# Clustered attention and two mixers on one core: mask rows of the first pair transposed early, transfers issued by SyncE, the other mask rows in eight pieces

## What is computed

```python
q_assign = np.argmax(np.einsum('bhsd,hcd->bhsc', q_n, c_n), axis=-1)
k_assign = np.argmax(np.einsum('bhsd,hcd->bhsc', k_n, c_n), axis=-1)
mask = q_assign[:, :, :, None] == k_assign[:, :, None, :]
scores = scale * np.matmul(q, k.transpose(0, 1, 3, 2))
scores = np.where(mask, scores, -1000000000.0)
attn = softmax(scores)
out = np.matmul(attn, v)
x = _moe_ref(x=out as (batch, token, head*dim), **moe_kwargs)
return _moe2_ref(x=x, **moe2_kwargs)
```

## Time and profile before

| | us |
|---|---|
| median of 3 runs | 792.31 (790.92 to 794.45) |
| the profiled execution | 793.93 |
| its span, first to last instruction | 792.0 |
| PE busy | 768.9 (97%) |
| DVE busy | 448.5 (57%) |
| ACT busy | 359.4 (45%) |
| POOL busy | 136.2 (17%) |
| preparation, to the last turning-back | 0 to 45 |
| first pair's tiles | 45 to 75 |
| rest of attention | 75 to 269 |
| mixers | 269 to 792 |

### The profile page before, as it was taken

The page is one execution under the profiler, slowest core; times in us unless marked ns, Lnnn a source line. Parts: engine busy times, 40 slices in busy tenths (PEclk is TensorE's granted clock), DMA queues, the critical chain, the costliest instruction groups (busy, mean ns, idle before and its releaser), DMA issues.

```text
span 792.0 us, 12875 instructions
## 1 busy us (share of the span) xinstructions
PE 768.9 (97%) x3985; PEld 661.3 (83%) x3985; DVE 448.5 (57%) x761; ACT 359.4 (45%) x740; POOL 136.2 (17%) x162
## 2 busy tenths in 40 slices
PE   6979999999999789999999999999999999999998
PEld 6968999999999668888888888888888888888886
DVE  4758999999999684333532353334254335334333
ACT  5547888888888524323332332332123233323321
POOL 1341332233228660000300040000300000000000
PEclk9979999999999999999999999999999999999999
DMA  8725444444441223332333323333003233332334
GB/s 289 184 82 135 111 105 119 104 120 102 121 101 49 74 87 93 105 98 87 97 90 106 89 83 119 84 101 96 11 1 107 93 93 92 95 106 84 102 105 174
DMA packets 82712, 81.08 MB, mean 102 GB/s; under 512 B 7296, under 2 KB 68864, under 8 KB 82688
## 3 DMA queue, kind: packets, MB, share of 16 engines
q1 hardware_dynamic: 81984, 79.00, 34.9%
q10 hardware_dynamic: 704, 1.77, 0.6%
HBM read 56.95 MB, written 4.72 MB: 78 GB/s over the span
## 4 chain that ended last, share of the span: by engine, by line
PE 63%; DVE 2%; ACT 0%; issue 0%
PE bank L958 29%; PE bank L967 29%; PE bank L945 2%; PE bank L926 2%; PE bank L909 1%; DVE kT_hi L1068 1%; DVE x L1086 0%; DVE x L1119 0%; DVE w_lo L1058 0%; DVE t L1077 0%; ACT qT_hi L1017 0%; DVE uT_lo L1063 0%
## 5 line engine op out<-in xcount | busy, mean ns | idle before, releaser
L1095 DVE SCALAR_TENSOR_TENSOR h_lo<-bank,h_hi 128x512 fp32r<-128x512 f32 x84 | 58.0, 691 | 259.3 <-ACT h_hi L1036 259.3
L1036 ACT ACTIVATE h_hi<-bank 128x512 fp32r<-128x512 f32 x84 | 50.2, 598 | 299.1 <-PE bank L958 299.1
L958 PE MATMUL bank<-uT_hi,w_hi 128*128 128x512 f32 x336 | 131.2, 391 | 0.0
L967 PE MATMUL bank<-w_hi,h_hi 128*128 128x512 f32 x336 | 131.1, 390 | 0.0
L958 PE MATMUL bank<-uT_hi,w_lo 128*128 128x512 f32 x336 | 130.8, 389 | 0.0
L967 PE MATMUL bank<-w_hi,h_lo 128*128 128x512 f32 x336 | 130.8, 389 | 0.0
L958 PE MATMUL bank<-uT_lo,w_hi 128*128 128x512 f32 x336 | 130.7, 389 | 0.0
L967 PE MATMUL bank<-w_lo,h_hi 128*128 128x512 f32 x336 | 130.7, 389 | 0.0
L572 DVE TENSOR_TENSOR pT_lo<-back,pT_hi 128x384 fp32r<-128x384 f32 x192 | 98.1, 551 | 8.1 <-ACT pT_hi L475 4.8
L475 ACT ACTIVATE pT_hi<-back 128x384 fp32r<-128x384 f32 x192 | 84.5, 496 | 38.2 <-PE back L709 35.7
L565 DVE TENSOR_REDUCE negmax<-front 128x1 f32<-128x768 f32 x96 | 91.2, 951 | 7.9 <-PE front L618 7.9
(11 more groups left out here) (123 smaller groups left out, 1051.9 us busy)
## 6 DMA issues: line engine op xcount, KB each, us to landing
w_raw<-in_moe_w_ch_dram SPq DMA_DIRECT2D x168, 256.0 KB, 2.8
Q<-qT_hi SPq DMA_DIRECT2D x64, 96.0 KB, 2.1
K<-kT_hi SPq DMA_DIRECT2D x64, 96.0 KB, 2.1
q_raw<-in_q_dram SPq DMA_DIRECT2D x8, 384.0 KB, 6.6
k_raw<-in_k_dram SPq DMA_DIRECT2D x8, 384.0 KB, 6.4
Q<-qT_lo SPq DMA_DIRECT2D x32, 96.0 KB, 2.1
K<-kT_lo SPq DMA_DIRECT2D x32, 96.0 KB, 2.1
v_raw<-in_v_dram SPq DMA_DIRECT2D x16, 192.0 KB, 2.8
```

Source lines behind the costliest of these rows:

```text
L958: last = nc.tensor.matmul(hid[par][:, :], w[par][:, kd, :], y[cc % 2][:, kd, :], start=(kd == 0 and m == 0), stop=(kd == KD - 1 and m == 2))
L967: last = nc.tensor.matmul(acc[k][:, :], y[par][:, k * P:(k + 1) * P], w[par][:, :], start=(start and m == 0), stop=(stop and m == 2))
L1036: nc.scalar.activation(h_hi[par][:, :], hid[par][:, :], ACT.Relu).then_inc(h_hi_made, 1)
L1095: nc.vector.scalar_tensor_tensor(out=h_lo[par][:, :], in0=hid[par][:, :], scalar=0.0, in1=h_hi[par][:, :].bitcast(F32), op0=ALU.max, op1=A ...
```

## The change

- **PE, preparation:** the two OH steps go. Two steps `("OHQ", 0, u)` come, six transposes each of only the first pair's 32 one-hot rows, one behind SB(2, queries) and one behind SA(2, keys). They take part in the alternation of `back[0]` and `back[1]`. `("S", 0, 0)` goes ahead of BACK of group 3 and S(1) comes behind it; BACK 3 waits for the low part of T(7,q).
- **DVE:** the row maximum of tile 0 (`MAX`) goes behind FIRST of group 2 and ahead of BEST of group 3.
- **ACT:** copies the OHQ steps into `ohq`, issues no DMA any more.
- **First pair:** the one-hot rows of both batch entries are transposed in eight pieces, behind S(2), T(0), S(3), T(1), S(4), T(2), and two behind S(5). Each batch entry has its own place in `x`.
- **SP:** the first eight raw loads, then the wait for three low parts; then each of the other eight loads is followed by three of the 24 head rows. Then both v loads, the mask rows of the first pair from `ohq` (four DMAs), U and V, the four stores of mask rows (each behind its copies), and the loop as before.

```diff
-            ohT = [x[:, 4 + n, 0:S] for n in range(2)]
+            ohT = [[x[:, 4 - 2 * b + n, 0:S] for n in range(2)] for b in range(B)]
+            ohq = [x[0:2 * C, GT * n:GT * n + GT, S:S + S // GT] for n in range(2)]
...
-        pe_steps += [sims[LAST][0], ("BACK", LAST - 1, 0), sims[LAST][1], ("OH", 0, 0), sims[LAST][2], ("OH", 0, 1),
-                     sims[LAST][3], ("BACK", LAST, 0)]
+        for u in range(2):
+            pe_steps.insert(pe_steps.index(("SB", LAST - 1, 0) if u == 0 else ("SA", LAST - 1, 1)) + 1, ("OHQ", 0, u))
+        pe_steps += [sims[LAST][0], ("BACK", LAST - 1, 0), sims[LAST][1], sims[LAST][2], sims[LAST][3],
+                     ("S", 0, 0), ("BACK", LAST, 0), ("S", 1, 0)]
...
-        back_T = [step for step in T_order if step != in_front]
-        place = {step: back[(n + 1) % 2] for n, step in enumerate(back_T)}
+        back_steps = [step for step in pe_steps if step[0] in ("T", "OHQ") and step != in_front]
+        place = {step: back[n % 2] for n, step in enumerate(back_steps)}
...
-        dve_steps += [("BEST", LAST - 1, 0), ("EQ", LAST - 1, 0), ("FIRST", LAST - 1, 0), ("BEST", LAST, 0), ("EQ", LAST, 0)]
+        dve_steps += [("BEST", LAST - 1, 0), ("EQ", LAST - 1, 0), ("FIRST", LAST - 1, 0), ("MAX", 0, 0), ("BEST", LAST, 0), ("EQ", LAST, 0)]
-        OH_PIECES = 4
-        OH_COPIES = 2 + OH_PIECES
+        OH_PIECES = 8
+        PIECES_AFTER = {("S", 2): (0,), ("T", 0): (1,), ("S", 3): (2,), ("T", 1): (3,), ("S", 4): (4,), ("T", 2): (5,),
+                        ("S", 5): (6, 7)}
...
+            for _, i, n in T_order[0:NPAIR]:
+                load_raw(i, n)
             sp.wait_ge(prep_lo, T_place["T", 0, 1])
-            head_rows(0, 0)
-            head_rows(0, 1)
+            for at, (_, i, n) in enumerate(T_order[NPAIR:]):
+                sp.wait_ge(raw_tr, T_place["T", i - PAIRS, n])
+                load_raw(i, n)
+                for row in range(3 * at, 3 * at + 3):
+                    head_row(0, row // 12, row % 12)
+            head_v(0, 0)
+            head_v(0, 1)
+            for u in range(2):
+                sp.wait_ge(ohq_copied, u + 1)
+                for j in range(2):
+                    sp.dma_start((Q2, K2)[u][j][D:D + C, :].rearrange("p (n c) -> p n c", n=GT).bitcast(F32),
+                                 ohq[u][j * C:(j + 1) * C, :, :]).then_inc(head_in[j], 16)
...
+            for b in range(B):
+                for u in range(2):
+                    store_onehots(b, u, 4 * b + 2 * u + 2)
             sp.wait_ge(prep_lo, 2 * NPAIR)
+            sp.wait_ge(oh_stored[0], 32)
             sp.wait_ge(oh_stored[1], 32)
...
-                elif kind == "OH":
-                    act.wait_ge(oh_tr, u + 1)
-                    mask_rows(u, ohT[u], place[kind, i, u][:, 0:S])
-                    act.wait_ge(oh_copied, u + 1)
-                    for j in range(2):
-                        act.dma_start((Q2, K2)[u][j][D:D + C, :].bitcast(F32),
-                                      ohT[u][j * C:(j + 1) * C, :]).then_inc(head_in[j], 16)
-                    act.dma_start(onehot_dram[u, 0:P, :], ohT[u]).then_inc(oh_stored[0], 16)
+                elif kind == "OHQ":
+                    act.wait_ge(ohq_tr, u + 1)
+                    mask_rows(u, ohq[u], place[kind, i, u][0:2 * C, 0:S].rearrange("p (n c) -> p n c", n=GT),
+                              2 * C).then_inc(ohq_copied, 1)
...
-                    if first_pair and t in (2, 3):
-                        onehot_piece(2 * t - 3)
+                    for m in PIECES_AFTER.get(("S", t + 2), ()) if first_pair else ():
+                        onehot_piece(m)
...
-                if (kind, i, u) in back_T[2:]:
+                if (kind, i, u) in back_steps[2:]:
+                    before, at, which = back_steps[back_steps.index((kind, i, u)) - 2]
...
+                b, u, half = m // 4, m // 2 % 2, m % 2
+                pe.wait_ge(oh_made, 2 * b + 2)
+                pe.wait_ge(oh_eq, LAST + 1)
+                wait(pe, oh_copied, m)
```

More of the change, by code:

```diff
@@ L223, in attention @@
         in_front = ("T", 0, 1)
-        back_T = [step for step in T_order if step != in_front]
-        place = {step: back[(n + 1) % 2] for n, step in enumerate(back_T)}
+        back_steps = [step for step in pe_steps if step[0] in ("T", "OHQ") and step != in_front]
+        place = {step: back[n % 2] for n, step in enumerate(back_steps)}
         place[in_front] = front[:, 2 * BANK:4 * BANK]
-        place["OH", 0, 0] = place["OH", 0, 1] = back[0]
+        assert place["T", NPAIR - 1, 1] is back[0]
         def sim_place(i, u):
@@ L276, in _, with head_row, head_v @@
             v_heads = v.rearrange("b h s d -> (b h) s d")
[L278 to L287, removed]
+            def head_row(g, j, n):
+                dst, src = ((Q1[j][0:D, :], hi[0]), (Q1[j][D:P, :], lo[0]), (K1[j][0:D, :], hi[1]), (K1[j][D:P, :], hi[1]),
+                            (Q2[j][0:D, :], hi[0]), (K2[j][0:D, :], lo[1]))[n // 2]
+                e = n % 2
+                sp.dma_start(dst[:, e * GW:(e + 1) * GW].bitcast(F32),
+                             src[e * D:(e + 1) * D, g, j * GW:(j + 1) * GW].bitcast(F32)).then_inc(head_in[j], 16)
+            def head_v(g, j):
                 wait(sp, v_ready[j], g)
@@ L306, in _ @@
                 for j in range(2):
-                    head_rows(g, j)
+                    wait(sp, scored, g * TPP + (NT * (j + 1) - TPP))
+                    for n in range(12):
+                        head_row(g, j, n)
+                    head_v(g, j)
                     head_onehots(g, j)
@@ L420, in exp, with mask_rows @@
                                      accum_out=sums[:, t % TPP:t % TPP + 1]).then_inc(exp_done, 1)
-            def mask_rows(u, dst, lead):
+            def mask_rows(u, dst, lead, rows=P):
                 if u == 0:
[L425 to L428, removed]
+                    return nc.scalar.activation(dst, lead, ACT.Relu, scale=MASKED, bias=masked[0:rows, :])
+                return nc.scalar.activation(dst, lead, ACT.Sign)
             for kind, i, u in pe_steps:
@@ L493, in body @@
                     high(t, 1)
-                    if first_pair and t in (1, 2):
-                        onehot_piece(2 * t - 2)
+                    for m in PIECES_AFTER.get(("T", t), ()) if first_pair else ():
+                        onehot_piece(m)
                 if last_pair:
@@ L558, in _ @@
                                             ALU.is_equal).then_inc(oh_eq, 1)
+                elif kind == "MAX":
+                    rowmax(0, i)
                 else:
@@ L588, in body @@
                 if first_pair:
[L589 to L590 removed]
+                    rowmax(0, 1)
                     first_link(LAST)
@@ L643, in _ @@
                     continue
+                if kind == "S":
+                    if i == 0:
+                        pe.wait_ge(oh_eq, LAST)
+                    else:
+                        pe.wait_ge(sim_copied, 2 * (LAST + 1))
+                    scores(0, i)
+                    continue
                 if kind == "BACK":
                     if i == LAST:
-                        pe.wait_ge(prep_lo, T_place["T", NPAIR - 1, 1])
+                        pe.wait_ge(prep_lo, T_place["T", NPAIR - 1, 0])
                     for n in range(2):
@@ L657, in _ @@
                 out = place[kind, i, u]
-                if kind == "OH":
-                    pe.wait_ge(prep_lo, T_place["T", NPAIR - 2, 1])
-                    wait(pe, oh_copied, u)
-                elif (kind, i, u) in back_T[2:]:
-                    pe.wait_ge(prep_lo, T_place[back_T[back_T.index((kind, i, u)) - 2]])
+                if (kind, i, u) in back_steps[2:]:
+                    before, at, which = back_steps[back_steps.index((kind, i, u)) - 2]
+                    if before == "T":
+                        pe.wait_ge(prep_lo, T_place[before, at, which])
+                    else:
+                        pe.wait_ge(ohq_copied, which + 1)
                 if kind == "T":
@@ L711, in body @@
                             last.then_inc(p_tr, 1)
-                        if first_pair and n in (1, 2):
-                            onehot_piece(2 * n - 2)
                     elif kind == "AV":
@@ L738, in body @@
                         last.then_inc(av_tr, 1)
+                    for m in PIECES_AFTER.get((kind, n), ()) if first_pair else ():
+                        onehot_piece(m)
             over_pairs(pe, body)
```

56 lines of the change are left out of this document (21 added, 35 removed).

## The result

The changed kernel takes 794.53 us (median of 17 runs, 792.81 to 796.53), the kernel before 792.44 in the runs beside it (17 runs, 789.67 to 796.06). The ratio is 1.0026, 95% interval 1.0014 to 1.0037: 2.1 us slower. That is inside the 0.5% that the prediction took as no change, but clear of noise and outside the range of the prediction (787.5 to 793.8). What was named as rival C decided it: the raw loads come late.

A forecast was written before the change was run, and what follows sets the result against it. TensorE, busy 97% of the 792.0 us span, was taken as the bound. Gap 3.0, bank waits -1.0, maximum +1.3, pieces and ScalarE -1.3 sum to 2.0 us gained: median 792.31 to 790.3 us, range 787.5 to 793.8.

The forecast's parts named there:

- rival C: Preparation: late raw loads land 2.4 to 4.6 us after they are wanted; far end 794.9 us; chance 9%.
- the one on the raw loads: Preparation: held-back loads shared with head rows on SyncE's queue land in 4.4 us, so none is late.
- The gap at BACK 3: Group 3's last turning-back: TensorE's wait for ScalarE's copy goes once SyncE issues the DMAs; gain 3.0 us.
- Bank waits: Preparation: TensorE waits about 0.8 and 0.4 us for low parts before T(6,k) and T(7,k); cost 1.0 us.
- The maximum: First pair's start: row maximum 0 ahead of group 3's maximum and compare, tile 2 near 45.8; gain 1.3 us.
- Pieces and ACT: First pair, tiles 2 to 5: eight pieces and waits for ScalarE's copies give back 1.3 us.
- The second pair: Chain from the last mask piece to the second pair's first score tile unchanged; wait of about 1.5 us stays.
- Rival B: First pair: the clock falls all the same, three rounds cost 3.3 us, giving 793.6 us; chance 12%.
- a clock of 0.50 anywhere after 14 us: Sign that the forecast is wrong and the clock falls all the same.

The follow-up runs named there:

- a1: The changed kernel with SyncE issuing all 16 raw loads first and the 24 head rows after them; ratio 0.9985 to the kernel before.
- a5: a3 and a4 together, plus the row maximum of tile 0 ahead of FIRST of group 2 on VectorE; ratio 0.9974 to the kernel before.
- a2: a1 with SyncE waiting for three low parts ahead of the last eight raw loads, no head rows between them; ratio 0.9986 to the kernel before.
- b3: b2 with SyncE's wait for the landed stores right ahead of each later pair's mask rows; 787.5 us, ratio 0.9930 to the kernel before.
- a3: a1 with VectorE making T(7,q)'s low part ahead of the maximum and compare of group 1; ratio 0.9972 to the kernel before.
- a4: a1 with SyncE's wait for the landed stores right ahead of each later pair's mask rows; 789.52 us, ratio 0.9961 to the kernel before.
- a6: The changed kernel with ScalarE issuing the last eight raw loads in pairs, SyncE the 24 head rows without a pause; ratio 1.0003 to the kernel before.
- b2: The kernel before with only ScalarE's six DMA issues of the OH steps moved to SyncE; ratio 0.9975 to the kernel before.
- b1: The kernel before with only SyncE's order changed: last eight raw loads held back, three head rows behind each; ratio 1.0075 to the kernel before.

## Why the prediction was wrong

**The step that failed** is the one on the raw loads: "I take 4.4, the row of the stretch in which the new loads run; then the sixth lands at 28.7 and none is late." Issue times were right, the landing was not: 4.0 us for the first, 8.1 for the last. The row was measured when the queue of loads was running out; it says nothing of loads and rows kept up together for 18 us. What the engines carry in each kind of traffic was left out. By the rows of the kernel before, a load of 384 KB takes 1.1 us of full engines (372 GB/s), and three head rows (288 KB) take 1.7 us of 0.70 of them (173 GB/s), 1.2 us of full ones. That is 2.3 of every 2.35 us, nearly full. Even this sum falls short: at the measured 235 GB/s of the mixture a load and three rows take 2.9 us, so the queue grows. What was late next was the load, not the bank.

**Rival C** had the place and the point from which it decides, and priced its far end at 4.6 us where 5.0 came (it gives 794.9 there; 794.5 was measured). Its mechanism was off in one half: the rows' issue never took 0.83 (at most 0.62; a load every 2.5 us, not 3.0); all of it was landing time. At 9% it was far too unlikely, and the range should have held its far end.

**The gap at BACK 3**: right, 3.0 us gone. **Bank waits**: hidden in the changed kernel behind the later loads, visible in a1 at the predicted 0.8 and 0.4. **The maximum**: in a1 tile 2 comes 26.2 us behind T(4,q), 26.0 predicted, and FIRST is what holds it, though a5 shows that freeing it brings nothing. **Pieces and ACT**: from tile 2 to tile 6 the walk has 12.2 us; it was 12.7 in the changed kernel, in a1 and in a2, 10.85 before. So the eight pieces and their waits give back 1.8, 0.5 more than I had. The kernel before runs 6.2 us of that stretch at the low clock; b3, with four pieces and 3.4 us of low clock, takes 9.75, so against it the eight pieces cost 2.9. **The second pair**: the chain and its wait of 1.5 us stand as forecast (14.86 us from score tile 6 against 14.84). So with the loads in time the sum was 2.0 where 1.7 is seen on the yardstick and 1.2 in the times.

**Rival B** (the clock): at 1.00 from 44 to 60 us in the changed kernel, and in a1, a3 and a5, as forecast. In a2, a4 and a6 it was at 0.50 for 3.4 us in the same stretch, for a4:

```profile
46.00:48.00 2.00, 1.90 (x10) 1.52 (x9) 0.34 (x2) 1.65 (x4) 1.95 (x2) 0.50 0.01 4
```

There it cost nothing: tile 2 to tile 6 took 12.69 us in a2 and a4 and 12.68 in a1. So with eight pieces my price of 3.3 us was wrong, since ACT's rounds leave PE time to be slow in. Elsewhere the low clock has a price: 1.5 and 1.6 us at the second pair in a2 and b2, and in b2 against b3, both with four pieces, 1.0 us for 5.8 instead of 3.4 us of it between tiles 2 and 6. The kernel before scatters with it too: of its 75 runs beside the experiments, the 15 with a mean granted clock of 0.989 have a median of 794.3 us, the 11 with 0.996 one of 790.6.

The forecast's evidence against B was one trace's luck. Around 270 us, where the clock stayed at 1.00 in the kernel before, PE is idle for the same 2.20 us in the changed kernel, and there the clock fell to 0.50 for 3.4 us (the row of 272 to 274 us above). So the sign "a clock of 0.50 anywhere after 14 us" came true, but at no cost: behind the second pair's first tile the two kernels take 717.0 and 717.2 us. The Trainium skill says that transposes don't count as busy time for the clock in the way that matmuls do (TensorE: Matmul & The Clock Gate, PE-mode transpose). These runs neither bear that out nor refute it: with the same order of work the clock fell in some runs and not in others.

## What to carry to other kernels

Ahead of shifting transfers between each other, add up the bytes per microsecond that the new order asks for, kind by kind, against the rate at which rows of the same kind had full DMA engines; a landing time read where a queue is running out is no price where it fills. A wait for landed stores belongs right ahead of the transfer that reads them, not ahead of the queue's other work. Undo the parts of a large change one by one: here moving six DMA issues (b2) brought as much alone as all of the change with its loads in time (a1), and the order of loads and rows (b1) lost more than that. The narrow steps, the early score tile and the eight pieces were only run together, so none of them has a price of its own here.

## What was not expected of the hardware

Loads from DRAM alone ran at 372 GB/s with full DMA engines; mixed with rows between on-chip tensors the engines were as full at 233 to 280, on one queue or on two. Two kernels with the same work around an idle time of 2.20 us of PE (near 270 us) came out of it with a granted clock of 1.00 and of 0.50. At the start six transposes took 1.5 us, nearly twice their later 0.82, while the granted clock read 1.00 (7 to 9 us of the changed kernel). Transposes of 32 weight columns took PE the same 0.82 us for six as those of 128.
